# Queries loaded into 64 rows with their rests made across rows, and the first feed-forward weights in single pieces a pair of heads

## The reference

```python
scores = scale * np.matmul(q, k.transpose(0, 1, 3, 2))      # scale = 1/8
mask = (rel >= 0) & (rel < 128)
scores = np.where(mask, scores + bias[None], -1e9)
attn = softmax(scores); x = np.matmul(attn, v)              # then tokens x 512
h = x @ w_in;  x = (h * (1 / (1 + np.exp(-1.702 * h)))) @ w_out
h = x @ w_in2; x = np.where(h >= 1, h, np.where(h <= -1, 0.0, (h + 1) ** 2 / 4)) @ w_out2
```

## Time and profile before

| | |
|---|---|
| median of 3 runs (lowest, highest) | 882.63 us (881.43, 884.73) |
| the profiled execution: its own time, its span | 883.84 us, 882.1 us |
| PE, DVE, ACT, POOL busy of the span | 859.3, 710.4, 536.6, 113.5 us |
| result of pair 0 and pair 15 written (start of L1553) | 25.2 us, 168.2 us |

### The profile page before, as it was taken

One profiled execution on the slowest core, in us unless ns is written; L12 is line 12 of the kernel. 1 busy time (PEld: TensorE's weight loads), 2 busy tenths in 40 slices (PEclk: granted clock), 3 DMA queues, 4 the chain that ended last, 5 costly groups with the idle time before them and its releaser, 6 DMA issues.

```text
span 882.1 us, 15505 instructions
## 1 busy us (share of the span) xinstructions
PE 859.3 (97%) x5746; PEld 852.8 (97%) x5746; DVE 710.4 (81%) x985; ACT 536.6 (61%) x788; POOL 113.5 (13%) x78
## 2 busy tenths in 40 slices
PE   7998889999999999999999999999999999999998
PEld 7998879999999999999999999999999999999998
DVE  6886788457798877677997987988989779889794
ACT  4875667566675565667754546676556576765431
POOL 3788487300000000000000000000000000000000
PEclk9999898999999999999999999999999999999999
DMA  8998692168766553677857465388554653788822
GB/s 204 241 259 227 174 249 81 42 262 283 281 237 213 203 212 129 244 257 278 315 204 282 160 223 179 146 305 304 211 203 169 237 192 141 273 288 293 310 81 72
DMA packets 63369, 191.17 MB, mean 217 GB/s; under 512 B 7488, under 2 KB 14400, under 8 KB 59456
## 3 DMA queue, kind: packets, MB, share of 16 engines
q1 hardware_dynamic: 63296, 190.18, 64.5%
HBM read 117.81 MB, written 72.35 MB: 216 GB/s over the span
## 4 chain that ended last, share of the span: by engine, by line
PE 86%; DVE 5%; POOL 4%; issue 2%; SPq 1%; ACT 1%; DMA 1%; DVEq 0%; POOLq 0%; ACTq 0%
PE ps L1041 79%; PE ps L1009 3%; PE ps L975 2%; POOL qk_hi L888 2%; PE ps L988 2%; POOL k_lo L884 1%; DVE wst L1572 1%; DVE probs L1540 1%; DVE qk_hi L1516 1%; DMA qk_raw<-qkT 1%; POOL w_first L908 1%; PE ps L1018 1%; SPq L568 1%; DVE heads_out L1553 1%; PE ps L1003 0%
## 5 line engine op out<-in xcount | busy, mean ns | idle before, releaser
L1041 PE MATMUL ps<-arena,w_first 128*128 128x384 f32 x1764 | 331.6, 336 | 0.9 <-ACT ps L1288 0.8
L1041 PEld LDWEIGHTS ps<-arena,w_first 128*128 128x128 f32 x1764 | 310.8, 188 | 2.4 <-issue 1.7
L1041 PE MATMUL ps<-arena,w_rest 128*128 128x384 f32 x1260 | 240.8, 337 | 0.9 <-ACT ps L1288 0.8
L1041 PEld LDWEIGHTS ps<-arena,w_rest 128*128 128x128 f32 x1260 | 220.1, 188 | 2.0 <-issue 1.7
L1645 DVE TENSOR_TENSOR arena<-raw_first,arena 128x768 fp32r<-128x768 f32 (+1 forms) x114 | 148.9, 1319 | 77.8 <-ACT arena L1260 77.8
L1260 ACT ACTIVATE arena<-raw_first 128x768 fp32r<-128x768 f32 (+1 forms) x120 | 132.0, 1117 | 45.6 <-DVE raw_first L1604 39.3
L1041 PE MATMUL ps<-w_rest,arena 128*128 128x256 f32 x945 | 132.5, 281 | 0.0
L1041 PEld LDWEIGHTS ps<-w_rest,arena 128*128 128x128 f32 x945 | 121.1, 189 | 0.1
L1041 PE MATMUL ps<-w_first,arena 128*128 128x256 f32 x567 | 88.0, 282 | 0.0
L1645 DVE TENSOR_TENSOR arena<-raw_rest,arena 128x1536 fp32r<-128x1536 f32 (+1 forms) x48 | 71.4, 1487 | 11.3 <-ACT arena L1260 11.2
L1041 PEld LDWEIGHTS ps<-w_first,arena 128*128 128x128 f32 x567 | 76.0, 189 | 0.0
(11 more groups left out here) (115 smaller groups left out, 975.0 us busy)
## 6 DMA issues: line engine op xcount, KB each, us to landing
gd<-g SPq DMA_DIRECT2D x24, 1536.0 KB, 6.1
raw_rest<-gd SPq DMA_DIRECT2D x32, 768.0 KB, 5.7
qk_raw<-qkT SPq DMA_DIRECT2D x60, 288.0 KB, 6.9
wst<-w_pairs SPq DMA_DIRECT2D x32, 512.0 KB, 6.5
raw_first<-gd SPq DMA_DIRECT2D x16, 768.0 KB, 6.1
yd<-ust SPq DMA_DIRECT2D x6, 1536.0 KB, 6.3
wd<-ust SPq DMA_DIRECT2D x4, 1536.0 KB, 9.3
raw_first<-yd SPq DMA_DIRECT2D x4, 1536.0 KB, 7.0
```

The costliest lines, as they stand in the source:

```text
L1041: last = nc.tensor.matmul(to, stationary, moving, start=start and n == 0, stop=n == len(steps) - 1, skip_group_check=True)
```

## The change

It has two parts.

**Queries once.** A head's keys and queries go to rows 0 to 63 as before, but rows 64 to 127 get the keys alone (288 KB and 144 KB in place of 288 KB twice). The query region of rows 64 to 127 of `qk_raw` is zeroed once by POOL at the start, and ACT and DVE wait for that before their first step. The rests of the queries are still written to rows 64 to 127 of `qk_hi`, now out of rows 0 to 63.

**Weights and first operands in pieces.** The work on w = 0, 1, 2 and on the first chunk is put at other heads (POOL) and steps (DVE, ACT); one piece of w = 0 goes from POOL to DVE, two of w = 1 from DVE to POOL, and SP loads w = 3 later.

```diff
-    def all_queries(tile, head):
+    def all_queries(tile, head, rows):
         at = (SEQ, TAIL)[head % 2]
-        return tile[DIM:P, head % SPLIT_RING, at:at + SEQ]
+        return tile[rows, head % SPLIT_RING, at:at + SEQ]
...
             wait_past(sp, qk_split[slot], splits(head - SPLIT_RING))
-            for half in range(2):
-                sp.dma_start(loaded(qk_raw, head)[half * DIM:(half + 1) * DIM], qkT[head]).then_inc(qk_in[slot], 16)
+            sp.dma_start(loaded(qk_raw, head)[UPPER], qkT[head]).then_inc(qk_in[slot], 16)
+            keys_from = SEQ * (head % 2)
+            sp.dma_start(keys(qk_raw, head)[LOWER], qkT[head, :, keys_from:keys_from + SEQ]).then_inc(qk_in[slot], 16)
...
                 load_first_x(1)
-            if q == 14:
-                load_weights(3)
         for q in range(PAIR_COUNT - X_STORE_LAG, PAIR_COUNT):
             store_pair(q)
+            if q == PAIR_COUNT - X_STORE_LAG:
+                load_weights(3)
...
                 pool.wait_ge(qk_split[slot], splits(head) - 1)
-                nc.gpsimd.tensor_tensor(all_queries(qk_hi, head), all_queries(qk_raw, head), f32(all_queries(qk_hi, head)),
-                                        ALU.subtract).then_inc(qk_split[slot], 1)
+                nc.gpsimd.tensor_tensor(all_queries(qk_hi, head, LOWER), all_queries(qk_raw, head, UPPER),
+                                        f32(all_queries(qk_hi, head, UPPER)), ALU.subtract).then_inc(qk_split[slot], 1)
             pool.wait_ge(qk_split[slot], splits(head))
...
+        for e in range(2):
+            nc.gpsimd.memset(qk_raw[LOWER, e::2, (SEQ, TAIL)[e]:(SEQ, TAIL)[e] + SEQ], 0.0).then_inc(raw_cleared, 1)
         split_first_keys()
...
             split_head(head)
-            if head in (11, 12, 13):
-                add_weights(0, head - 11)
-            if head in (14, 15, 16):
-                split_weights(0, head - 14)
-            if head in (25, 26, 28, 29):
-                split_operand((A11, S1, S2, A12)[(25, 26, 28, 29).index(head)])
+            if head == 11:
+                add_weights(0, 0)
+            if head == 13:
+                add_weights(0, 1)
+                add_weights(0, 2)
+            if head in (15, 17):
+                split_weights(0, (15, 17).index(head))
+            if head in (23, 25):
+                split_weights(1, (23, 25).index(head))
+            if head in (21, 27, 29, 31):
+                split_operand((A11, S1, S2, A12)[(21, 27, 29, 31).index(head)])
         sum_s3()
...
         act.wait_ge(cleared, CLEARED)
+        act.wait_ge(raw_cleared, 2)
         act.wait_ge(distance_in, 16)
...
                 copy_pair(q)
-            if m in (30, 45, 70):
-                round_both((30, 45, 70).index(m))
-            if m in (55, 59, 64, 65, 77, 79):
-                round_operand(0, (55, 59, 64, 65, 77, 79).index(m))
+            if m in (30, 46):
+                round_weights((30, 46).index(m), 0)
+            if m in (32, 53):
+                round_weights((32, 53).index(m), 1)
+            if m in (44, 62, 67, 69, 77, 79):
+                round_operand(0, (44, 62, 67, 69, 77, 79).index(m))
+            if m == ALL_STEPS:
+                round_both(2)
...
                 dve.wait_ge(qk_rounded, head - 1)
-                nc.vector.tensor_tensor(all_queries(qk_hi, head), all_queries(qk_raw, head), f32(all_queries(qk_hi, head)),
-                                        ALU.subtract).then_inc(qk_split[slot], 1)
+                nc.vector.tensor_tensor(all_queries(qk_hi, head, LOWER), all_queries(qk_raw, head, UPPER),
+                                        f32(all_queries(qk_hi, head, UPPER)), ALU.subtract).then_inc(qk_split[slot], 1)
...
-        def add_weights(w):
-
-            w_staged(dve, w)
-            dve.wait_ge(w_ready, 3 * nth(w))
-            for step in range(3):
+        def add_weights(w, steps=(0, 1, 2)):
+
+            if 0 in steps:
+                w_staged(dve, w)
+                dve.wait_ge(w_ready, 3 * nth(w))
+            for step in steps:
                 if step:
...
-        def split_weights_part(w, step):
-
-            dve.wait_ge(w_rounded, 2 * nth(w) + (1 if step == 0 else 2))
-            if step == 0:
-                to, a, hi = made_first(w)[:, 1], w_b11(w), made_first(w)[:, 0]
-            else:
-                some = slice(3 * step - 3, 3 * step)
-                to, a, hi = made_rest(w)[:, some, 1], w_others(w)[:, some], made_rest(w)[:, some, 0]
-            nc.vector.tensor_tensor(to, a, f32(hi), ALU.subtract).then_inc(w_ready, 1)
+        def split_last_weights(w):
+
+            dve.wait_ge(w_rounded, 2 * nth(w) + 2)
+            dve.wait_ge(w_ready, 3 * nth(w) + 2)
+            nc.vector.tensor_tensor(made_rest(w)[:, 3:6, 1], w_others(w)[:, 3:6], f32(made_rest(w)[:, 3:6, 0]),
+                                    ALU.subtract).then_inc(w_ready, 1)
...
         dve.wait_ge(cleared, CLEARED)
+        dve.wait_ge(raw_cleared, 2)
         round_first(0)
...
                 round_head(m + 1)
-            if m == 43:
-                add_weights(1)
-            if m in (46, 48, 51):
-                split_weights_part(1, (46, 48, 51).index(m))
-            if m in (58, 63):
-                sum_operand(0, S1 if m == 58 else S2)
-            if m == 66:
-                add_weights(2)
+            if m in (41, 71):
+                split_last_weights(0 if m == 41 else 1)
+            if m in (46, 51):
+                add_weights(1, (0,) if m == 46 else (1, 2))
+            if m in (61, 66):
+                sum_operand(0, S1 if m == 61 else S2)
+            if m in (76, ALL_STEPS):
+                add_weights(2, (0,) if m == 76 else (1, 2))
             for head in range(SPLIT_RING, 2 * PAIR_COUNT):
...
                     round_head(head)
```

More of the change, by code:

```diff
@@ L67 @@
 TAIL_AT = (SEQ + 4 * P, 0)
+UPPER, LOWER = slice(0, DIM), slice(DIM, P)
 ZEROS_AT = (2 * SEQ, 0)
@@ L179, in build @@
     cleared = sem("cleared")
+    raw_cleared = sem("raw_cleared")
     warm_ready = sem("warm_ready")
@@ L285, in piece_keys, with piece_queries @@
         return tile[:, 1, KEYS_AT[1]:keys_at] if first else tile[:, 1, keys_at:WIDTH]
-    def piece_queries(tile, e, first):
-        return piece(tile, 0, first)[DIM:P, 1] if e == 0 else all_queries(tile, 1)
+    def piece_queries(tile, e, first, rows):
+        return piece(tile, 0, first)[rows, 1] if e == 0 else all_queries(tile, 1, rows)
     def piece_lo(e, first):
@@ L566, in load_piece @@
                 source_piece = qkT[1, :, 0:SEQ + FIRST_COLS] if first else qkT[1, :, SEQ + FIRST_COLS:2 * SEQ]
-            for half in range(2):
-                sp.dma_start(piece(qk_raw, e, first)[half * DIM:(half + 1) * DIM],
-                             source_piece).then_inc(first_in[e] if first else qk_in[e], 16)
+            source_keys = qkT[e, :, SEQ * e:SEQ * (e + 1)]
+            source_keys = source_keys[:, 0:FIRST_COLS] if first else source_keys[:, FIRST_COLS:SEQ]
+            landed = first_in[e] if first else qk_in[e]
+            sp.dma_start(piece(qk_raw, e, first)[UPPER], source_piece).then_inc(landed, 16)
+            sp.dma_start(piece_keys(qk_raw, e, first)[LOWER], source_keys).then_inc(landed, 16)
         def load_operands(head):
@@ L1507, in split_rest @@
                                     ALU.subtract).then_inc(qk_split[0], 1)
[L1508 to L1509 removed]
+            nc.vector.tensor_tensor(piece_queries(qk_hi, 0, False, LOWER), piece_queries(qk_raw, 0, False, UPPER),
+                                    f32(piece_queries(qk_hi, 0, False, UPPER)), ALU.subtract).then_inc(qk_split[0], 1)
         def round_head(head):
```

6 lines of the change are left out of this document (2 added, 4 removed).

## The result

The changed kernel takes **871.63 us** (median of 4 runs, 870.08 to 874.07) against 883.13 us for the kernel before beside it (4 runs, 881.43 to 884.73): a ratio of 0.9873, 95% interval 0.984 to 0.9905. The forecast was 865, the range 861 to 876. The waits that the change was aimed at went; of the gain of 18.3 us that the sum gave, the profiled executions show 13.3 (883.84 to 870.50).

A forecast was written before the change was run, and what follows sets the result against it. PE bounds the kernel, with 21.6 us lost between the first 16 pairs. From 883.84: -21.6 between pairs, -1.3 start, +1.6 head 20, +2.4 DVE, +0.3 POOL, +0.3 ACT = 865.5, stated as 865; own range 861.5 to 869, wider range 861 to 876.

The forecast's parts named there:

- rival A: DVE waits 2.4 us or more for head 20, PE's clock falls, a gap costs 6 us: 870 to 876; chance 0.20.
- Pieces on POOL, the wait at head 17: Two pieces no longer precede head 17's rests on POOL, which come up to 4.0 us earlier; PE's 2.62 us wait goes.
- Start: Fewer bytes to load at the start, so DVE waits less for early heads: 1.3 us gained, between 0 and 2.
- Zeroing: Two POOL memsets come first while DVE and ACT wait: cost 0 to 1.1 us, taken as 0.
- Rests across rows: POOL's rests from rows 0 to 63 into 64 to 127: same 1.42 us assumed, at most twice that.
- rival B: POOL's rests across rows are slow and the kernel slower: about 7 us slower at twice the length, 890; chance 0.06.
- Head 20: Its load queues behind w = 2's on SP; DVE stands still 0.9 us, the next pair is 1.6 us late.
- Pieces on DVE: Pieces placed behind the bias of steps 5q+1, priced at length less DVE's 1.3 us spare: 2.4 us, bound 5.
- on POOL, 0.3: The largest piece makes a pair of heads 8.2 us on POOL against 8.06, once or twice: 0.3 us for lateness.
- Nothing here reaches the 2.4 us after which the clock fell: Said of the head 20 delay: waits stay below the idle time after which PE's granted clock drops to 1.2 GHz.
- ACT's round at m = 80: The rounding of w = 2 on ACT can hold its last copy of probabilities: 0.3 us.
- Rival C: Waits move: seven DVE pieces in eight pairs cost as the 2.03 us one did: 876 to 880; chance 0.07.

The follow-up runs named there:

- queries_once: The kernel before with the first part of the change alone (queries loaded to 64 rows, zeroing, rests across rows), feed-forward pieces as before: 881.07 us, ratio 0.9979.
- w2_later: The changed kernel with the load of w = 2 put behind the loads of heads 20 and 21 in SP's order: 869.92 us, ratio 0.9857.
- dve_small: The changed kernel with DVE's pieces of w = 0, w = 1 and two operand sums cut to 8 columns a block, POOL's whole: 868.76 us, ratio 0.9838.
- pool_small: The changed kernel with POOL's pieces of w = 0, w = 1 and three operands cut to 8 columns a block, DVE's whole: 865.33 us, ratio 0.9803.
- new_pieces: The kernel before with the second part of the change alone: new places of the pieces, queries still loaded twice: 874.14 us, ratio 0.9905.
- one_port_late: The changed kernel with DVE's casts from head 8 on as tensor_scalar with a row-sum output, expected not to use the second port: 867.46 us, ratio 0.9821.

## Why the prediction was right, and where its sum was off

- **The range and the direction held, the range in part by luck.** The waits of the earlier trace rows are gone or down to 1.5 us, and with them the pairs of 12 and 15 us. But 871.6 lies outside the 861.5 to 869 of the forecast itself. It is inside 861 to 876 because that range also takes in rival A, and rival A is not what happened: the cast of head 20 waited 0.41 us and not 2.4. Two of the prediction's own signs point the same way: pair 15 was written at 155.15 and not near 150, and PE's clock did not stay at 1.00. In the last step of the sum, 865.5 less 1.2 is 864.3, not 865.
- **Pieces on POOL, the wait at head 17: right.** PE does not wait for POOL there. `queries_once`, which keeps the old places, still has it, 2.63 us.
- **Start: 1.84 us, forecast 1.3**, within its bounds. **Zeroing: 0, right.** Both memsets (partitions x elements) are over at 2.8 us, and the first cast waits for its DMA until 4.63:

```profile
0.74 2.05 POOL L933 MEMSET qk_raw<- 64x1152 f32 x2 [0.29 <-POOLq L1950]
```

- **Rests across rows: the same 1.41 us, right**; rival B falls. Reading rows 0 to 63 and writing rows 64 to 127 costs nothing extra. The Trainium skill's rule on POOL's eight cores ("GPSIMD Engine Reference", Architecture) does not show in the time of this instruction.
- **Head 20: right in kind, smaller.** The cast waited 0.41 us, forecast 0.9; the trace of `w2_later` puts it at 0.5 us for the pair, forecast 1.6. The third part of the chain, the clock, did not follow: it stayed at 1.00 in that pair.

```profile
84.99 0.76 DVE L1533 CAST qk_hi<-qk_raw 128x1152 fp32r<-128x1152 f32 x1 [0.41 <-DMA qk_raw<-qkT]
```

- **Pieces on DVE, 2.4 us, and on POOL, 0.3: the terms that were mis-sized.** Of the 10.9 us over pace, 0.5 is the last pair and the prediction had 4.6 for everything else; it was 10.4. `dve_small` and `pool_small` put 3 to 4 us on DVE's pieces and about 8 on POOL's (each alone; they overlap, since together they could give at most the 10.4). The step that failed is "a piece of 1.62 us made a pair of 8.42 ... its length less the 1.3 spare". DVE's 6.75 busy us of a pair at full pace held 0.8 us of being shut out (two free casts are 1.5 us; the pair at 39.46 has 0.75 + 1.56), and in a pair with a POOL piece its casts stand still for 2.4 us. POOL's piece, which was charged only with POOL's own lateness, takes DVE's time. The signs were in the rows: the cast of 1.37 us in the earlier trace rows beside one of 0.76 in the earlier trace rows, and POOL's maximum of 2.0 us for an instruction of 1.4 in the earlier trace rows.
- **The subtractions of w = 1 on DVE, at m = 46 and 51: a term that the sum left out.** Rival C counts seven pieces, the 2.4 us are made of five. The two of m = 51 stand in the pair of 9.91, the longest of all, 1.85 us over pace; together they took 2.78 us, where one alone takes 0.42 us in the feed-forward part:

```profile
95.93 2.78 DVE L1590 TENSOR_TENSOR wst<-wst 128x256 f32<-128x256 f32 x2
```

- **"Nothing here reaches the 2.4 us after which the clock fell": wrong in what it concluded.** No single wait did, but the clock fell all the same, behind the pair of m = 51 and not at head 20. The stretches of 2 us from 98 on in the changed kernel, PE busy for 1.59 and 1.03 of 2.00 us, then a mean clock of 0.60 and 0.55, that is, the lower level of 1.2 GHz for most of it:

```profile
98.00:100.00 2.00, 1.59 (x14) 1.38 (x14) 2.00 (x9) 0.94 (x2) 0.62 (x2) 1.00 0.30 114
100.00:102.00 2.00, 1.03 (x10) 0.85 (x8) 1.93 (x10) 1.89 (x3) 1.92 (x2) 1.00 0.51 96
102.00:104.00 2.00, 2.00 (x14) 2.00 (x14) 1.96 (x7) 2.00 (x6) 1.43 (x2) 0.60 1.01 354
104.00:106.00 2.00, 2.00 (x12) 2.00 (x12) 0.90 (x5) 0.31 (x1) 1.65 (x2) 0.55 1.05 237
```

  The length of the waits does not settle it. In `w2_later` PE is busy for 1.58 and 1.03 us of the same two stretches, and the clock stays at 1.00. A single wait of 1.50 us left it at 1.00 in the changed kernel (up to 82.86), one of 1.57 in `new_pieces` did not.

- **The rest of the program: right**, what follows the last pair takes 713.55 us. **ACT's round at m = 80**, charged at 0.3 us, shows nowhere: the last pair takes 8.55, and 8.56 before.
- **Rival C, "the waits move", came nearest in mechanism**: four pairs cost 1.75 to 1.85 us over pace, as the 1.7 of the piece of 2.03 us had. It reckoned with seven of them and with A's gap too, which stayed small.

What stays open: why pairs with two pieces of 768 columns take 0.1 us less than the sum, the one of 9.91 takes 0.1 more than its 9.81, and those with one piece take 0.2 to 0.5 more, what makes the clock fall at waits of 1 to 1.5 us in one execution and not in another, and why the loads of head 20 took longer to land in `one_port_late`. The order in which waiting instructions get the port was not tried.
